# Another order of the attention bursts in the steady slots: turning k with row_0, turning x with the last level, four slots left empty

## What is computed

```python
for t in range(S):
    cur = np.einsum('bhd,bhe->bhde', u[None] * kt, vt)
    y[:, :, t] = np.einsum('bhd,bhde->bhe', rt, state + cur)
    state = wt[:, :, :, None] * state + np.einsum('bhd,bhe->bhde', kt, vt)
```

## Time and profile before

| | |
|---|---|
| median of 3 runs | 997.16 us (996.25 to 998.93) |
| the profiled execution | 996.8 us; its span, from the first to the last instruction, 995.0 us |
| TensorE busy, products (PE) | 975.1 us, 98% of the span, 9722 products |
| TensorE busy, weight loads (PEld) | 800.8 us, 80% |
| VectorE busy (DVE) | 589.9 us, 59% |
| ScalarE busy (ACT) | 502.1 us, 50% |
| granted TensorE clock | 1.000 over the span |
| DMA | 61.67 MB, mean 62 GB/s |

### The profile page before, as it was taken

How to read it: one execution, slowest core, us unless ns; L and a number is a source line. 1 busy time by engine, 2 the same in 40 slices (tenths; PEclk the granted TensorE clock), 3 DMA queues, 4 the chain that set the end, 5 groups by cost and what they waited for, 6 DMA issues and landing times.

```text
span 995.0 us, 22373 instructions
## 1 busy us (share of the span) xinstructions
PE 975.1 (98%) x9722; PEld 800.8 (80%) x9722; DVE 589.9 (59%) x919; ACT 502.1 (50%) x895; POOL 48.2 (5%) x44
## 2 busy tenths in 40 slices
PE   8899999999999999999999999999999999999998
PEld 6788887788888888888888888888888888888886
DVE  7787878888888888878433545333334334333332
ACT  3555444444545454363546766444444445544543
POOL 6930000000000000000000000000000000000000
PEclk9999999999999999999999999999999999999999
DMA  8722312222220222031151100000100000000000
GB/s 296 258 100 71 117 33 110 66 80 81 97 81 1 81 97 80 2 112 50 48 177 47 32 32 1 32 33 1 32 32 32 9 24 32 33 1 0 32 1 32
DMA packets 24689, 61.67 MB, mean 62 GB/s; under 512 B 2448, under 2 KB 6928, under 8 KB 24592
## 3 DMA queue, kind: packets, MB, share of 16 engines
q1 hardware_dynamic: 24592, 60.25, 17.1%
HBM read 50.80 MB, written 9.44 MB: 61 GB/s over the span
## 4 chain that ended last, share of the span: by engine, by line
PE 82%; DVE 1%; ACT 0%; issue 0%; ACTq 0%; DVEq 0%
PE down_banks L681 38%; PE work_banks L681 24%; PE first_up_bank L681 20%; PE work_banks L796 1%; PE work_banks L876 1%; DVE att L1262 0%; DVE att L1235 0%; DVE att L1265 0%; ACT r_nat L989 0%; DVE att L1296 0%; DVE g_lo L1398 0%; DVE ynat L1348 0%; DVE att L1311 0%; DVE att L1298 0%; DVE att L1272 0%
## 5 line engine op out<-in xcount | busy, mean ns | idle before, releaser
L681 PE MATMUL down_banks<-g_hi,wout_lo 128*128 128x512 f32 (+1 forms) x624 | 244.2, 391 | 0.8 <-DVE g_lo L1398 0.8
L681 PE MATMUL down_banks<-g_hi,wout_hi 128*128 128x512 f32 (+1 forms) x624 | 235.4, 377 | 0.0
L681 PE MATMUL down_banks<-g_lo,wout_hi 128*128 128x512 f32 (+1 forms) x624 | 235.2, 377 | 0.0
L1398 DVE TENSOR_TENSOR g_lo<-scratch,g_hi 128x512 fp32r<-128x512 f32 (+1 forms) x192 | 128.1, 667 | 110.8 <-ACT g_hi L989 110.7
L989 ACT CAST g_hi<-scratch 128x512 fp32r<-128x512 f32 (+1 forms) x192 | 116.0, 604 | 100.5 <-PE down_banks L681 70.5
L1090 ACT ACTIVATE scratch<-first_up_bank,consts 128x512 f32<-128x512 f32 (+1 forms) x88 | 57.2, 650 | 196.6 <-PE first_up_bank L681 109.2
L681 PEld LDWEIGHTS down_banks<-g_hi,wout_lo 128*128 128x128 f32 x624 | 117.4, 188 | 27.1 <-DVE g_lo L1398 1.2
L681 PEld LDWEIGHTS down_banks<-g_hi,wout_hi 128*128 128x128 f32 x624 | 117.5, 188 | 23.2
L681 PEld LDWEIGHTS down_banks<-g_lo,wout_hi 128*128 128x128 f32 x624 | 117.7, 189 | 20.6
L681 PE MATMUL first_up_bank<-x_hi,win_lo 128*128 128x512 f32 (+1 forms) x336 | 127.9, 381 | 0.3 <-DVE x_lo L1403 0.2
L1493 DVE SCALAR_TENSOR_TENSOR scratch<-scratch,work_banks 128x512 f32<-128x512 f32 x72 | 49.5, 688 | 132.7 <-ACT scratch L1162 132.7
(11 more groups left out here) (127 smaller groups left out, 1141.1 us busy)
## 6 DMA issues: line engine op xcount, KB each, us to landing
att<-rT_dram SPq DMA_DIRECT2D x12, 512.0 KB, 3.5
att<-kT_dram SPq DMA_DIRECT2D x12, 512.0 KB, 4.4
att<-wT_dram SPq DMA_DIRECT2D x12, 512.0 KB, 5.9
r_nat<-rN_dram SPq DMA_DIRECT2D x12, 384.0 KB, 4.3
k_nat<-kN_dram SPq DMA_DIRECT2D x12, 384.0 KB, 4.7
att<-vN_dram SPq DMA_DIRECT2D x12, 384.0 KB, 6.0
x_dram<-r_nat SPq DMA_DIRECT2D x18, 256.0 KB, 2.3
ynat<-x_dram SPq DMA_DIRECT2D x6, 768.0 KB, 4.3
```

Source lines behind the costliest of these rows:

```text
L681: return nc.tensor.matmul(out, lhsT, rhs, start=start, stop=stop, **kw)
L1398: nc.vector.tensor_tensor(g_of(g_lo, F), sum_of(F), g_of(g_hi, F).bitcast(F32), ALU.subtract).then_inc(glo_ready, 1)
```

## The change

The two tables and `DIAGONAL` are written anew. In a steady tile (c = 2 and 3), slot by slot:

| slot | before | after |
|---|---|---|
| 0 | last g0 | turn_k g0, row_0 g0 |
| 1 | turn_k g0 (values g1) | pair 0 g1 |
| 2 | pair 0 g1 | row_1 g0 |
| 3 | row_0 g0 | pair 2 g1 |
| 4 | pair 2 g1 | none (values g1) |
| 5 | row_1 g0 | pair 4 g1 |
| 6 | pair 4 g1 | none (keys g0, g1) |
| 7 | turn_x g0 (keys g0, g1) | last g1, turn_x g0 |
| 8 | last g1 (bonus g0, g1) | turn_k g1, row_0 g1 |
| 9 | turn_k g1 (sums g0) | pair 0 g0 of the next chunk |
| 10 | pair 0 g0 of the next chunk | row_1 g1 |
| 11 | row_0 g1 | pair 2 g0 |
| 12 | pair 2 g0 | none (bonus g0, g1) |
| 13 | row_1 g1 | pair 4 g0 |
| 14 | turn_x g1 (sums g1, values g0) | turn_x g1, last g0 |
| 15 | pair 4 g0 | none (sums g0, g1, values g0) |

Tile 1 keeps its first three slots (pair 4 g0, last g0, pair 0 g1), has turn_k and row_0 of group 0 in slot 3, pair 2, row_1 and pair 4 in slots 4 to 6 (with values g1 in 4 and keys in 6), and follows the new table from slot 7 on. In tile 4 the steps of the next chunk fall away: pair 0, pair 2 and pair 4 of group 0 and its last.

Turned k of both groups goes to work banks 2 and 3, and `attend` no longer waits for the copied k in these tiles. VectorE does the suffixes of a pair at one place, behind the outputs of the next slot.

```diff
--- before.py
+++ after.py
@@ -65,15 +65,14 @@
 STAGES_FIRST = [("level", l) for l in range(NL)]
 STAGES_MIXED = STAGES_FIRST[:4] + [("pair", 4), ("level", NL - 1)]
 STAGES = [("pair", 0), ("pair", 2), ("pair", 4), ("level", NL - 1)]
-WORK_TILE_1 = {0: [("pair", 0, 0, 4)], 1: [("last", 0, 0)], 2: [("pair", 0, 1, 0)], 3: [("turn_k", 0, 0)],
-               4: [("pair", 0, 1, 2)], 5: [("row_0", 0, 0)], 6: [("pair", 0, 1, 4)], 7: [("row_1", 0, 0)],
-               8: [("last", 0, 1), ("turn_x", 0, 0)]}
-WORK = {0: [("last", 0, 0)], 1: [("turn_k", 0, 0)], 2: [("pair", 0, 1, 0)], 3: [("row_0", 0, 0)],
-        4: [("pair", 0, 1, 2)], 5: [("row_1", 0, 0)], 6: [("pair", 0, 1, 4)], 7: [("turn_x", 0, 0)],
-        8: [("last", 0, 1)], 9: [("turn_k", 0, 1)], 10: [("pair", 1, 0, 0)], 11: [("row_0", 0, 1)],
-        12: [("pair", 1, 0, 2)], 13: [("row_1", 0, 1)], 14: [("turn_x", 0, 1)], 15: [("pair", 1, 0, 4)]}
-DIAGONAL = {1: [("values", 1, 1)], 7: [("keys", 2, 0), ("keys", 2, 1)], 8: [("bonus", 2, 0), ("bonus", 2, 1)],
-            9: [("sums", 2, 0)], 14: [("sums", 2, 1), ("values", 2, 0)]}
+WORK_TILE_1 = {0: [("pair", 0, 0, 4)], 1: [("last", 0, 0)], 2: [("pair", 0, 1, 0)], 3: [("turn_k", 0, 0), ("row_0", 0, 0)],
+               4: [("pair", 0, 1, 2)], 5: [("row_1", 0, 0)], 6: [("pair", 0, 1, 4)]}
+WORK = {0: [("turn_k", 0, 0), ("row_0", 0, 0)], 1: [("pair", 0, 1, 0)], 2: [("row_1", 0, 0)], 3: [("pair", 0, 1, 2)],
+        5: [("pair", 0, 1, 4)], 7: [("last", 0, 1), ("turn_x", 0, 0)], 8: [("turn_k", 0, 1), ("row_0", 0, 1)],
+        9: [("pair", 1, 0, 0)], 10: [("row_1", 0, 1)], 11: [("pair", 1, 0, 2)], 13: [("pair", 1, 0, 4)],
+        14: [("turn_x", 0, 1), ("last", 1, 0)]}
+DIAGONAL = {4: [("values", 1, 1)], 6: [("keys", 2, 0), ("keys", 2, 1)], 12: [("bonus", 2, 0), ("bonus", 2, 1)],
+            15: [("sums", 2, 0), ("sums", 2, 1), ("values", 2, 0)]}
 X2_SLOTS = (8, 9, 10)
 WQ = 512
 W2Q = KT * FF // 4
@@ -177,7 +176,7 @@
 
             if k >= 2:
                 ds = work_banks[:, 2, b % 2 * HP * D:(b % 2 + 1) * HP * D]
-                return work_banks[:, 2 - 2 * (b // 2) + b % 2, :], work_banks[:, 0, :], ds, work_banks[:, 2 + b % 2, :]
+                return work_banks[:, 2 + b % 2, :], work_banks[:, 0, :], ds, work_banks[:, 2 + b % 2, :]
             if (k, b) == (0, 0):
                 return y_bank, up_bank[0], y_bank, down_bank[0]
             if (k, b) == (0, 1):
@@ -347,8 +346,8 @@
             c, f, _ = SLOTS[F]
             if not 1 <= c < NC - 1:
                 return []
-            table = WORK_TILE_1 if c == 1 and f in WORK_TILE_1 else WORK
-            return [(what, c + 1 + ahead_, *rest) for what, ahead_, *rest in table[f] if c + 1 + ahead_ < NC]
+            table = WORK_TILE_1 if c == 1 and f <= max(WORK_TILE_1) else WORK
+            return [(what, c + 1 + ahead_, *rest) for what, ahead_, *rest in table.get(f, []) if c + 1 + ahead_ < NC]
 
         def diagonal_at(F):
 
@@ -800,7 +799,7 @@
             def attend(k, b):
 
                 g = b // 2
-                if k > 0 or b >= 2:
+                if k == 1 or k == 0 and b >= 2:
                     pe.wait_ge(kt_copied, k * B + b + 1)
                 if k > 0:
                     pe.wait_ge(state_ready, (k - 1) * B + b + 1)
@@ -1035,8 +1034,7 @@
 
                 act.wait_ge(kt_filled, k * B + 2 * g + 2)
                 act.wait_ge(ds_filled, k * 2 * B + 4 * g)
-                first = 2 - 2 * g
-                copy(later_k_turned[:, :].rearrange("p (b n) -> p b n", b=2), work_banks[:, first:first + 2, :])\
+                copy(later_k_turned[:, :].rearrange("p (b n) -> p b n", b=2), work_banks[:, 2:4, :])\
                     .then_inc(kt_copied, 2)
 
             def both_x_hi_of(k, g):
@@ -1448,10 +1446,6 @@
             def layer1_slot(F):
                 c, f, _ = SLOTS[F]
                 work = work_at(F)
-                before = [what for what, *_ in work_at(F - 1)]
-                for what, k, g, *l in work_at(F - 1):
-                    if what == "pair" and l[0] < 4 and before == ["pair"] and not work[0][0].startswith("row"):
-                        suffixes(k, g, l[0] + 2)
                 if work and work[0][0] == "pair":
                     pair_slot(F, *work[0][1:])
                     for what, k, g in diagonal_at(F):
@@ -1461,7 +1455,7 @@
                     if what in ("row_0", "row_1"):
                         output(k, 2 * g + (what == "row_1"))
                 for what, k, g, *l in work_at(F - 1):
-                    if what == "pair" and l[0] < 4 and work[0][0].startswith("row"):
+                    if what == "pair" and l[0] < 4:
                         suffixes(k, g, l[0] + 2)
                 for what, k, g, *l in work_at(F + 1) if F + 1 < LAYER_1 else ():
                     if what == "pair" and l[0] == 0:
```

## The result

The changed kernel takes 1009.74 us (median of 6 runs, 1008.56 to 1013.28) against 998.04 us for the kernel before in the same series (6 runs, 996.25 to 1007.57). The ratio is 1.0113, with a 95% interval of 1.0086 to 1.0139: slower, as forecast, but by 11.7 us where 8.4 were forecast, and 1.2 us outside the range of 1000 to 1008.5. A second series gave 1.0102 (1.0076 to 1.0129), 1009.44 against 999.38 us.

A forecast was written before the change was run, and what follows sets the result against it. TensorE, busy throughout tile 3, was taken as the bound. New waits of 7.9 and 2.2 us, less 0.45, 0.5 and 0.7, gave +8.4 us on 996.8: 1005.2 us, range 1000 to 1008.5.

The forecast's parts named there:

- Row_1 behind pair 0: Slots 3 and 11: the next pair burst waits 1.31 us for VectorE's state, six times over tiles 1 to 4, 7.9 us.
- Pair 4 in front of an empty slot: Slot 6 of tiles 2 to 4: the down product waits for VectorE's late g_lo, 3 x 0.72 = 2.2 us.
- The waits of turn_x: Tiles 2 to 4: 0.15 us each, already waited for g_lo behind turn_x's burst, goes: -0.45 us.
- The up bank: Empty slots: ScalarE reads the single up bank in time for the next up product, 0.6 us of cover, cost 0.
- Merged bursts: 14 more slots with two bursts back to back on TensorE: each saves about 0.05 us, 0.7 us in all.
- (b): Rival: each of the 14 merged bursts saves 0.4 us, half the turning, 5.6 instead of 0.7; 1000.3 us; 8%.
- (c): Rival: in the 14 merged bursts TensorE hides the turning completely, 11.1 us instead of 0.7; 994.8 us, faster; 4%.
- Tile 1: Moved diagonal parts and waits in tile 1: -0.8 + 0.2 + 0.2 - 0.12 = -0.5 us.
- (a): Rival: the state is in time for the pair bursts, so the 7.9 us of waits fall away; 997.3 us; 10%.
- (d): Rival: TensorE's clock falls to 1.2 GHz in nine slots with a new wait, +38 us, 1043 us; 2%.
- The sum for tiles 1 to 4: All terms of the change together: 7.9 + 2.2 - 0.45 - 0.5 - 0.7 = +8.4 us.
- the base of the sum: The profiled execution's 996.8 us, 0.4 under the median of 997.16, to which the 8.4 us were added.

## Why the prediction came out as it did

- **Row_1 behind pair 0: right.** Forecast 6 waits of 1.31 us, 7.9 us; measured 6 of 1.26 to 1.29, 7.7 us. Undone by moving the state, 7.3 us came back.
- **Pair 4 in front of an empty slot: right.** 3 x 0.73 us against 3 x 0.72.
- **The waits of turn_x (-0.45 us): right**; in slots 7 and 14 of the changed kernel no down product waits for g_lo. The up bank was read in time and the other empty slots cost nothing.
- **Merged bursts: mis-sized.** Forecast -0.7 us (0.05 each), measured 0 to 0.03 each, some -0.2 us in all. Rivals (b) and (c) are out.
- **Tile 1: nearly right.** The down product in slot 2 waited 0.83 us less, as forecast, slots 6 and 8 got waits of 0.20 and 0.28 us (forecast 0.2 and 0.2). By tile I was wrong: I had forecast +0.7 for tile 1 and +1.7 for tile 4 and they grew by 1.35 and 1.08 us. The last of the next chunk, 0.81 us, moves from slot 0 of a tile to slot 14 of the tile before; tile 1 gains one and tile 4 loses one, and I had overlooked that. The sum isn't touched.
- **Rivals (a) and (d): out.** Every state wait stands where it was put, and the clock is 1.00 in tiles 1 to 4 behind all transposes and all waits. The rule of the Trainium skill that was cited (TensorE: Matmul & The Clock Gate, Part 4: PE-mode transpose) isn't borne out here: no fall in these tiles, where bursts of 6 to 8 transposes stand beside waits of up to 1.29 us.
- **The sum for tiles 1 to 4: +8.4 forecast, +8.9 measured**, the difference being mostly the merges.
- **The step that failed is the base of the sum and the width of the range.** "The profiled execution took 996.8 us ... 0.4 under the median of 997.16": I took this one execution as typical. It was one of the fastest, with no fall of the clock in tile 0 and the shortest time behind tile 5, so the sum was added to the best case; 12 executions of the kernel before with a mean clock of 1.000 took 996.8 to 998.0 us. The longer series of the kernel before gives 999.4 and 999.6 us (29 and 23 runs), over 2 us more, and 999.4 + 8.9 = 1008.3. The range was built from unknown costs of the change alone and had nothing for what lies outside the changed slots: up to 6 us from tile 0's clock in some executions, up to 2.1 us behind tile 5. In the first series the changed kernel's six runs all had mean clocks of 0.991 to 0.996. Against the second series' own baseline the forecast would have been 999.4 + 8.4 = 1007.8 us, 1.6 under the measured 1009.4 and inside a range moved up by as much. Of the 4.5 us between 1005.2 and 1009.74, 0.5 are the sum's and 4.0 the base's. What makes a single execution's clock fall, and the spacing behind tile 5, stay open.

## What to carry to other kernels

Where one engine is busy without a gap, a new order of the same work is worth what waits it removes, and here there were next to none; back-to-back bursts of different shape saved nothing. Cost it by following the helper engine's chain from the event that starts it to the signal that the full engine needs, in the new order; here two instructions at the end of a slot, which had been done 0.80 us before they were needed, made 7.3 of the 8.9 us, and moving them ahead of two others gave these back. And take the base and the width of a forecast from the spread of the runs, not from the profiled one, even where only three runs are shown.

## What was not expected of the hardware

- TensorE's granted clock falls to its lower level (1.2 GHz) in tile 0 in some executions and not in others of the same kernel. Behind the same idle time of 2.1 us, near 100 us, it fell for 3.4 or 6.8 us in 8 of 13 profiles, and stayed at 1.00 in 5 (the burst at 101.77 of the first profile has it). Near 15 us, behind an idle time of 1.4 to 1.5 us that all have too, it fell in 4. The longest fall, 10.2 us from 36.7 us on in the changed kernel's first profile, came behind idle times of 0.8 and 0.7 us. A chain of nine 128x256 products, 1.05 us from the first start to the last, takes 1.88 us at the lower level. In the changed kernel's first profile, with two falls, tile 1 started 5.9 us later than in the profile of before, which had none; in the second of the kernel before, with one, 1.5 us later.
- Runs of 128x512 products without any wait, the same instructions, proceed at one of two spacings, 232.4 or 233.3 to 233.4 ns a product, with the clock at 1.00 throughout. Each is kept for a stretch of 16 slots (66.9 or 67.2 us), and which stretches are slow differs between profiles of one program: 472.4 to 474.5 us for the same 2034 products.
